# Two places of one planned kernel: VectorE's emptying of the first down-projection ahead of its split of the next x, and block 0's last down-projection units moved ahead of block 1

## The reference, cut to what matters

```python
def _attn_ref(x, weight_gen):          # x [2, 4096, 192], weight_gen [2, 4096, 8, 7]
    ...                                # w = softmax over the 7 taps, per token and head
    out = np.einsum('bshk,bskhg->bshg', w, x_unf)   # 7-tap causal mix of tokens
def _moe_ref(x, w_gate, w_val, w_out, rms_g):       # 192 -> 1536 -> 192
    xn = x / np.sqrt(np.mean(x * x, axis=-1, keepdims=True) + 1e-06) * rms_g
    g = xn @ w_gate
    return (g * (1.0 / (1.0 + np.exp(-g))) * (xn @ w_val)) @ w_out
def _moe2_ref(x, w_in, w_out):                      # 192 -> 2048 -> 192
    h = x @ w_in
    return (h * (1.0 / (1.0 + np.exp(-1.702 * h)))) @ w_out
```

## Time and profile before

| | us |
|---|---|
| three runs | 1347.87, 1348.52, 1350.25 (median 1348.52) |
| profiled execution, its own time | 1349.41 |
| profiled execution, span from first to last instruction | 1347.6 |
| TensorE matmul busy | 1244.0 (92% of the span) |
| VectorE busy | 789.5 (59%) |
| ScalarE busy | 667.5 (50%) |
| GpSimd busy | 97.8 (7%) |
| mean granted TensorE clock | 0.972 of full |

### The profile page before, as it was taken

How to read it: one execution, slowest core, us unless ns; L and a number is a source line. 1 busy time by engine, 2 the same in 40 slices (tenths; PEclk the granted TensorE clock), 3 DMA queues, 4 the chain that set the end, 5 groups by cost and what they waited for, 6 DMA issues and landing times.

```text
span 1347.6 us, 28916 instructions
## 1 busy us (share of the span) xinstructions
PE 1244.0 (92%) x11968; PEld 1117.8 (83%) x11968; DVE 789.5 (59%) x1218; ACT 667.5 (50%) x1194; POOL 97.8 (7%) x108
## 2 busy tenths in 40 slices
PE   0878898998989989898998989999898998989998
PEld 0767887988879988787998879899887988988898
DVE  6878467383754738467383755738466383753442
ACT  3243554545555545554545555544454545555454
POOL 7872000000000000000000000000000000000000
PEclk9989899999999989999999999989999999999999
DMA  5331000010000001000010000001000000000000
GB/s 139 92 107 33 1 17 30 5 42 2 17 30 17 30 1 45 1 17 31 5 43 1 20 27 17 31 1 45 2 16 30 17 31 1 14 1 13 1 2 25
DMA packets 14625, 33.69 MB, mean 25 GB/s; under 512 B 1828, under 2 KB 7842, under 8 KB 14496
## 3 DMA queue, kind: packets, MB, share of 16 engines
q1 hardware_dynamic: 14496, 31.85, 7.4%
HBM read 25.55 MB, written 6.29 MB: 24 GB/s over the span
## 4 chain that ended last, share of the span: by engine, by line
PE 78%; ACT 6%; DVE 5%; issue 4%; ACTq 0%; DVEq 0%
PE up_ps L775 34%; PE acc L775 27%; PE up_ps L779 9%; PE acc L779 8%; ACT hidden L542 2%; ACT L542 1%; ACT h_hi L552 1%; DVE shifted L677 1%; DVE y_f L679 1%; DVE hidden L733 1%; DVE x_lo L650 1%; ACT x_f L490 1%; DVE x_rest L658 1%; ACT silu L536 1%; ACT x_f L496 1%
## 5 line engine op out<-in xcount | busy, mean ns | idle before, releaser
L742 DVE TENSOR_TENSOR h_lo<-hidden,h_hi 128x512 fp32r<-128x512 f32 x448 | 314.9, 703 | 437.4 <-ACT h_hi L552 437.3
L552 ACT CAST h_hi<-hidden 128x512 fp32r<-128x512 f32 x448 | 278.3, 621 | 259.7 <-DVE hidden L733 252.0
L775 PE MATMUL acc<-out_w,h_hi 64*128 64x384 f32 x1024 | 316.9, 368 | 50.3 <-DVE y_f L679 49.3
L779 PE MATMUL acc<-out_w,h_hi 64*128 64x384 f32 x1024 | 316.9, 368 | 0.0
L542 ACT ACTIVATE hidden<-up_ps 128x512 f32<-128x512 f32 x256 | 152.5, 596 | 276.0 <-PE up_ps L779 275.8
L775 PE MATMUL acc<-out_w,h_lo 64*128 64x192 f32 x1024 | 261.2, 255 | 0.0
L779 PE MATMUL acc<-out_w,h_lo 64*128 64x192 f32 x1024 | 261.1, 255 | 0.0
L775 PE MATMUL up_ps<-x_hi,up_w 64*128 64x512 f32 x800 | 254.4, 398 | 6.6 <-DVE x_hi L648 6.6
L779 PE MATMUL up_ps<-x_hi,up_w 64*128 64x512 f32 x800 | 254.8, 398 | 0.0
L775 PEld LDWEIGHTS acc<-out_w,h_hi 64*128 64x128 f32 x1024 | 196.4, 192 | 57.2 <-issue 52.4
L775 PE MATMUL acc<-h_hi,out_w 64*128 64x512 f32 x576 | 196.9, 395 | 6.9 <-DVE y_f L679 4.5
(11 more groups left out here) (106 smaller groups left out, 3238.1 us busy)
## 6 DMA issues: line engine op xcount, KB each, us to landing
x_win<-in_x_dram SPq DMA_DIRECT2D x14, 960.0 KB
out_dram<-out_sb SPq DMA_DIRECT2D x15, 384.0 KB, 2.3
stage<-in_moe_w_out_dram SPq DMA_DIRECT2D x13, 192.0 KB, 2.5
logits<-in_weight_gen_dram SPq DMA_DIRECT2D x16, 112.0 KB, 2.0
stage<-in_moe_w_in_dram SPq DMA_DIRECT2D x4, 256.0 KB, 2.8
stage<-in_moe_w_in_dram SPq DMA_DIRECT2D x8, 128.0 KB, 2.8
stage<-in_moe_w_val_dram SPq DMA_DIRECT2D x3, 256.0 KB, 3.8
stage<-in_moe_w_val_dram SPq DMA_DIRECT2D x6, 128.0 KB, 2.7
```

Source lines behind the costliest of these rows:

```text
L552: nc.scalar.copy(h_hi[:, u % 4, :], hidden[:, u % 2, :]).then_inc(hi_ready, 1)
L742: nc.vector.tensor_tensor(h_lo[:, u % 4, :], hidden[:, u % 2, :], h_hi[:, u % 4, :].bitcast(F32), ALU.subtract).then_inc(lo_ready, 1)
L775: return nc.tensor.matmul(ps, w[TOP], data[TOP], start=start, stop=stop)
L779: return nc.tensor.matmul(ps, w[LOW], data[LOW], start=start, stop=stop)
```

## The change

The slot constants change. VectorE's `split_x` runs at slot 17 rather than slot 14, so behind `empty_y_rest` of slot 15. The emptying of block 0's accumulator runs at slot 1 of block 1 rather than slot 2, on ScalarE and VectorE. (For group 1 `split_x` stays after slot 11 of block 0.) On TensorE, units 10 and 11 of block 0 no longer ride in steps 0 and 1 of block 1. Unit 10 is issued at block 0's end, its first two top matmuls beside the last low ones of unit 9, its other three alone; then come the turn of x for group 1, unit 10's low matmuls alone, and unit 11's top matmuls alone. Unit 11's low matmuls run beside the first top matmuls of block 1's step 0. No instruction that computes is added or removed.

```diff
-    EVAC_O, EVAC_Y0, SQUARE, SPLIT_Y, X_T, SPLIT_X, EVAC_Y, LAST_Y = 1, 2, 8, 8, U1 - 1, U1 + 2, U1 + 3, U1 + 4
+    EVAC_O, EVAC_Y0, SQUARE, SPLIT_Y, X_T, EVAC_Y, LAST_Y, SPLIT_X = 1, 1, 8, 8, U1 - 1, U1 + 3, U1 + 4, U1 + 5
...
                 if down is None:
                     low_pair(i, p, 3 + k)
                 elif k == 0:
-                    low_pair(i, p, 8)
+                    if p is not None:
+                        low_pair(i, p, 8)
                 else:
                     low_down1(*down, k - 1)
...
                     if u >= 2:
                         before = step(i, u, before, (i, u - 2))
-                    elif i == 1:
-                        before = step(i, u, before, (0, U1 - 2 + u))
                     else:
                         before = step(i, u, before)
                     if i > 1 and u < 2:
...
                 if i == 0:
                     for k in range(6):
                         low_tail(before, k)
-                    before = None
-                if i < GROUPS - 1:
+                        if k >= 4:
+                            top_down1(0, U1 - 2, k - 4)
+                    for k in range(2, 5):
+                        top_down1(0, U1 - 2, k)
+                    turn_x(1)
+                    for k in range(5):
+                        low_down1(0, U1 - 2, k)
+                    for k in range(5):
+                        top_down1(0, U1 - 1, k)
+                    before = (0, None, (0, U1 - 1))
+                elif i < GROUPS - 1:
                     turn_x(i + 1)
```

## The result

The changed kernel takes 1283.61 us (median of four runs, 1283.08 to 1283.96) where the kernel before takes 1348.19 on the same chips: a ratio of 0.9519, 95% interval 0.9503 to 0.9536. The profiled execution took 1283.08 us with a span of 1281.3, against 1349.41 and 1347.6, so the two traces differ by 66.3 us.

A forecast was written before the change was run, and what follows sets the result against it. TensorE's work plus its holes, mainly fourteen 3.50 us waits for y_f and the low clock behind them, bound the kernel. 34.3 + 26.4 + 0 + 5.5 = 66.2 us gained, giving a median of 1282.3 us, range 1276 to 1294.

The forecast's parts named there:

- the two large terms: Blocks 1 to 14: 34.3 us from shorter waits for y_f and 26.4 us from low-clock stretches gone.
- the third: Block 0 to block 1: a gain of 5.5 us, bounds 1 and 7.5.
- Fourteen waits: TensorE's waits for y_f in blocks 1 to 14 fall from 3.50 to 1.05 us: gain 34.3 us.
- The clock: Low-clock stretches behind the fourteen waits vanish: gain 26.4 us; the rival that it still falls had 0.10.
- the 28 that the prediction named as a sign: In the profile after, TensorE's busy time about 28 us less for the same matmuls.
- The rule that spoke against it: Frequent small idles between matmul groups make TensorE's clock swing; the clock gain would be 0 rather than 26.4 us.
- The moved split: split_x at slot 17, between h_lo of slots 17 and 18: cost 0; rival that it is in the way 0.06.
- Block 0: Block 0 to block 1: new TensorE order and earlier y_f gain 5.5 us, bounds 1 and 7.5.
- the 1.4 us of low clock: Behind the wait up to 106.79: TensorE would not enter the low stretch of some 3 us, 1.4 us lost.
- the 1.5 taken back: Block 0's gain of 7.0 reduced by 1.5 us, as VectorE's next work meets GpSimd's weight splits.
- The 13 matmuls: From about 86.5, 13 matmuls of units 10, 11 and x take 5.2 us, covered by the wait up to 92.30.
- low matmuls "long done": Low matmuls of the first down-projection are long done, so shifted follows h_lo of slot 14 at once; 1.05 us wait left.

The follow-up runs named there:

- The last experiment: Against the changed kernel, VectorE empties acc_rest one slot earlier, ahead of h_lo of slot 14, and split_x is back at slot 14: 1266.67 us, ratio 0.9391.
- the version at 1266: Against the changed kernel, VectorE empties acc_rest one slot earlier, ahead of h_lo of slot 14; split_x stays at slot 17: 1266.40 us, ratio 0.9392.

## Why the prediction was right

The forecast was 1282.3 us with a range of 1276 to 1294, and 1283.6 was measured. The sum of the gains was 66.2; the two profiled executions differ by 66.3 and the medians by 64.6, as the profiled execution of the kernel before lay 1.2 us above its median and that of the changed kernel 0.5 below. The agreement of sum and difference to 0.1 us is partly luck; the two large terms are right by their mechanism, the third by errors that cancel.

- *Fourteen waits.* 1.05 us were forecast from block 15's 1.44 us from h_lo to y_f and the hand-over, and 1.06 to 1.07 came. 34.2 us, forecast 34.3. The row that carried this was of a block without the split in the old kernel.
- *The clock.* Between the cuts the same matmuls are busy 1079.23 - 1053.04 = 26.2 us less, forecast 26.4. The 0.46 us per microsecond at the low level holds in the experiments: a fall behind 2.12 us of wait costs 1.57 us for some 3.4 us at that level. Over the whole span TensorE's busy time fell by 25.9 us and not by the 28 that the prediction named as a sign, since ahead of the first cut it rose by 0.3 (98.99 to 99.33 us).
- *The rule that spoke against it.* The Trainium skill, TensorE: Matmul & The Clock Gate, section "A second HAM failure mode: psum-queue depth-cycling", has short idles lower the clock when they are frequent. The waits of 1.06 us, one in 76 us, did not lower it in 14 of 14, nor did those of 1.40. Waits that come much closer together were not tried, so the rule is not refuted; it made no difference in this kernel.
- *The moved split.* Cost 0, as forecast: h_lo of slot 18 starts at 152.11 and TensorE has no wait for it; from 140 to 1212 us its only waits are those for y_f, 15.1 us. The last experiment shows more than the forecast said: slot 14 is as good as slot 17, as long as the emptying is ahead of the split.
- *Block 0.* 5.5 us forecast; the cuts give 5.9 less the 0.4 from ahead of 92.30, 5.5, and the kernel without this part is 5.8 slower in the median. Its terms were a little off and made up for each other. The restart behind y_f came at 101.38 (forecast 101.2), which is 5.0 us earlier once the 0.4 are taken off, not 5.6. Of the 1.4 us of low clock and the 1.5 taken back, 0.5 us of gain is what was measured from there to block 1's stop (41.50 us for 42.00), forecast -0.1. The 13 matmuls fitted ahead of the wait for x, of which 2.19 us are left. (The prediction says that all 20 matmuls of units 10 and 11 run one at a time. In the order written 13 do: two run beside unit 9's last ones and five beside block 1's first. Its sum does not rest on this.) The later restart follows the clock: its low stretch ends at 97.6 and not at 96.25, 5.8 us behind the restart for x and not 4.0. Seven traces here have the same order and the same slot for block 0. From the first matmul that reads x_rest (91.87 in the changed kernel) to the restart behind y_f it takes 9.5 us in the three with 5.7 to 5.8 us of low clock between them, 8.9 in the two with 3.8 to 4.0, and 8.0 to 8.1 in the two with 2.6 to 2.7. The forecast's 101.2 is 8.9 us behind 92.30. So this term moves by up to 1.5 us with where the clock's low stretch falls in an execution, and no run tells why it falls where it does.

What the prediction did not see is the version at 1266: it named h_lo of slot 14 as what y_f is late behind, and stopped there, although low matmuls "long done" meant that VectorE could have emptied ahead of it.

## What to carry to other kernels

Where an in-order engine both frees something that TensorE waits for and prepares something that is read much later, put the freeing first, ahead even of a regular step whose result has slack; the place of the preparation is then free. A hole in TensorE's work of two to three and a half microseconds cost half to two thirds as much again here through the clock, so the last microseconds of such a wait are worth more than their length, and cutting it to 1.4 us already took all of the clock's part. Lengths between 1.4 and 2.1 us were not tried. A block at the edge of the loop that lacks the suspect step is the cheapest experiment there is: it stands in the old trace.

## What the runs showed of the hardware that was not expected

- The same wait of TensorE, 2.12 us with the same work before and behind it, was followed by the low clock in eleven blocks and not in three; 2.89 us in twelve of fourteen, 3.50 us in fourteen of fourteen, 1.06 and 1.40 us in none. What decides between blocks is not shown here.
- A wait of TensorE costs about 0.1 us more than the idle time that the profile counts for it, also at the full clock (76.31 - 75.16 - 1.06 = 0.09 and 76.65 - 75.16 - 1.40 = 0.09), because matmuls overlap: without a wait the next starts 0.16 us after a matmul that is counted as 0.25 us long.
- Beside GpSimd's weight splits, most of VectorE's instructions whose inputs all lie in SBUF (the engines' shared buffer) take longer, those that read PSUM (where TensorE's accumulators lie) do not. In the trace of the kernel before, the eleven h_lo that lie wholly beside them take 0.88 to 1.79 us and all others 0.69 at most; with one input, a cast of x_rest takes up to 1.49 us for 0.41. After the change, in block 1, with two rows of GpSimd:

```profile
105.30 0.94 DVE L624 TENSOR_TENSOR mixed<-x_win,probs 128x768 f32<-128x768 f32 x1
106.17 0.98 DVE L742 TENSOR_TENSOR h_lo<-hidden,h_hi 128x512 fp32r<-128x512 f32 x1
107.08 1.77 DVE L624 TENSOR_TENSOR tap<-x_win,probs 128x768 f32<-128x768 f32 x1
108.77 0.67 DVE L733 TENSOR_TENSOR hidden<-silu,up_ps 128x512 f32<-128x512 f32 x1
...
106.70 1.34 POOL L416 TENSOR_TENSOR out_w<-stage,out_w 128x384 fp32r<-128x384 f32 x1
108.10 1.12 POOL L409 CAST out_w<-stage 128x384 fp32r<-128x384 f32 x1
```

The product that reads the accumulator (L733) keeps its 0.67 us between two tap products, of which the next took 1.76 as well; without GpSimd beside them they take 0.95. The transfers do not explain it: in the kernel before, the DMA engines were 1% busy around the h_lo of 1.79 us at 101.89, and the h_lo at 76.17, with them 96% busy and GpSimd idle, took 0.68.
